# One transfer each for v, the sums and the reciprocals, a softmax chain spread over three periods, and finer waits into the second GEMM

## What is computed

```python
scores = cap * tanh((q @ k.T) / sqrt(64) / cap)      # batch 2, heads 12, seq 448, head_dim 64
attn = exp(scores - max) / (sum + 1e-9)
x = attn @ v                                         # then laid out as 896 x 768
h = x @ w_in                                         # 768 x 2048
x = maximum(0.01 * h, h) @ w_out                     # 2048 x 768
xn = x / rms(x) * rms_g
out = (silu(xn @ w_gate) * (xn @ w_val)) @ w_out2    # 768 x 1536, 1536 x 768
```

## Time and profile before

| | us |
|---|---|
| median of 3 runs | 644.47 (642.46 to 645.29) |
| the profiled execution | 639.19 |
| its span, first to last instruction | 637.1 |
| PE busy | 609.0 (96%) |
| DVE, POOL, ACT busy | 280.9, 203.8, 161.4 |
| mean granted clock of TensorE | 0.989 of full speed |

### The profile page before, as it was taken

The page is one execution under the profiler, slowest core; times in us unless marked ns, Lnnn a source line. Parts: engine busy times, 40 slices in busy tenths (PEclk is TensorE's granted clock), DMA queues, the critical chain, the costliest instruction groups (busy, mean ns, idle before and its releaser), DMA issues.

```text
span 637.1 us, 7470 instructions
## 1 busy us (share of the span) xinstructions
PE 609.0 (96%) x2988; PEld 529.8 (83%) x2988; DVE 280.9 (44%) x383; ACT 161.4 (25%) x227; POOL 203.8 (32%) x124
## 2 busy tenths in 40 slices
PE   4987999899999997999999999999999999999998
PEld 3543555389999996999999999999999999999998
DVE  3274655388888785033331236445434454110000
ACT  5773766223233231001111023112111111100000
POOL 1020000035445453144342343536454352332000
PEclk9997999899999998999999999999999999999999
DMA  6134343324333333021111121212221220023000
GB/s 202 36 86 106 77 121 89 90 70 124 99 118 107 103 121 108 34 66 34 67 56 36 50 74 48 77 50 75 54 95 51 74 74 1 26 75 125 37 26 37
DMA packets 33314, 47.76 MB, mean 75 GB/s; under 512 B 18176, under 2 KB 21504, under 8 KB 33280
## 3 DMA queue, kind: packets, MB, share of 16 engines
q1 hardware_dynamic: 33280, 47.29, 24.9%
HBM read 44.44 MB, written 2.80 MB: 74 GB/s over the span
## 4 chain that ended last, share of the span: by engine, by line
PE 91%; DVE 3%; issue 2%; ACT 2%; DMA 1%; POOL 1%; SPq 1%; DVEq 0%
PE ps L690 28%; PE ps L670 19%; PE ps L644 18%; PE ps L733 13%; PE ps L626 8%; PE ps L608 3%; PE ps L630 2%; PE ps L612 1%; ACT probs L355 1%; DVE g_lo L484 1%; DVE x_norm L460 1%; ACT probs L349 1%; DMA qk_raw<-in_qk 1%; POOL act_lo L322 0%; DVE qk_lo L435 0%
## 5 line engine op out<-in xcount | busy, mean ns | idle before, releaser
L297 POOL TENSOR_TENSOR w_lo<-w_raw,w_hi 128x768 fp32r<-128x768 f32 (+1 forms) x68 | 132.9, 1954 | 341.9 <-DVE w_hi L473 341.9
L473 DVE CAST w_hi<-w_raw 128x768 fp32r<-128x768 f32 (+1 forms) x68 | 39.5, 582 | 190.6 <-issue 128.2
L690 PE MATMUL ps<-x_hi,w_hi 128*128 128x448 f32 x288 | 82.0, 366 | 0.0
L690 PE MATMUL ps<-x_lo,w_hi 128*128 128x448 f32 x288 | 81.8, 365 | 0.0
L690 PE MATMUL ps<-x_hi,w_lo 128*128 128x448 f32 x288 | 81.8, 365 | 0.0
L626 PE MATMUL ps<-probs,v_ones 128*128 128x448 f32 x144 | 61.4, 579 | 10.4 <-issue 7.8
L644 PE MATMUL ps<-x_hi,w_hi 128*128 128x448 f32 x192 | 70.3, 366 | 0.5 <-POOL w_lo L297 0.5
L644 PE MATMUL ps<-x_lo,w_hi 128*128 128x448 f32 x192 | 70.1, 365 | 0.0
L644 PE MATMUL ps<-x_hi,w_lo 128*128 128x448 f32 x192 | 70.1, 365 | 0.0
L626 PEld LDWEIGHTS ps<-probs,v_ones 128*128 128x128 f32 x144 | 28.6, 204 | 38.8 <-issue 38.6
L484 DVE TENSOR_TENSOR g_lo<-g_full,g_hi 128x448 fp32r<-128x448 f32 x32 | 60.8, 1904 | 0.0
(11 more groups left out here) (84 smaller groups left out, 834.8 us busy)
## 6 DMA issues: line engine op xcount, KB each, us to landing
w_raw<-in_w_in SPq DMA_DIRECT2D x32, 384.0 KB, 3.0
w_raw<-in_w_out SPq DMA_DIRECT2D x12, 512.0 KB, 3.5
qk_raw<-in_qk SPq DMA_DIRECT2D x12, 480.0 KB, 4.3
w_raw<-in_w_gate SPq DMA_DIRECT2D x12, 384.0 KB, 3.0
w_raw<-in_w_val SPq DMA_DIRECT2D x12, 384.0 KB, 2.9
v_raw<-in_w_out SPq DMA_DIRECT2D x12, 384.0 KB, 3.0
recip_row<-recips SPq DMA_DIRECT2D x24, 112.0 KB, 2.9
v_ones<-in_v SPq DMA_DIRECT2D x24, 96.0 KB, 3.1
```

Source lines behind the costliest of these rows:

```text
L297: pool.tensor_tensor(w_lo[u % 2][:, 0:n], w_raw[u % 2][:, 0:n], w_hi[u % 2][:, 0:n].bitcast(F32), ALU.subtract).then_inc(w_lo_done, 1)
L473: dve.tensor_copy(w_hi[u % 2][:, 0:n], w_raw[u % 2][:, 0:n]).then_inc(w_hi_done, 1)
L690: last = pe.matmul(ps[:, 4 * fp + 2 * s + b, 0:S], w[s][:, c * 128:(c + 1) * 128], x[:, (b * KD + c) * S:(b * KD + c + 1) * S], start=(c = ...
```

## The change

**v, sums, reciprocals.** v lies in columns 0 to 63 of every block of `v_ones`, for both heads, and is loaded by one transfer a pair instead of four. The results of both heads then lie on partitions 0 to 63 and the sums of both on partitions 64 to 127. `keep_x` copies 65 partitions (64 of results and one of sums), one transfer spreads the sums of both heads, and one loads 64 partitions by 896 reciprocals. `normalise` reads both heads from partitions 0 to 63 and writes head 1 to partitions 64 to 127.

**The order.** In period p DVE does `split_qk(p + 2)`, `reciprocal(p - 1)`, `normalise(p - 2)` and then `keep_x(p)`. `normalise(10)` and `reciprocal(11)` stand behind `leaky(0)` of GEMM 1 and `normalise(11)` behind `g_lo(2)`. SP stores and loads back the reciprocals of pair p - 1 in period p, and v is loaded two pairs ahead.

**GEMM 2.** For the first output tile PE waits before each of the 16 blocks f for `g_lo` of that block, and no longer before the first block for the last but one.

The diff:

```diff
--- before.py
+++ after.py
@@ -77,7 +77,7 @@
         v_ones = [buf(f"v_ones{s}", (2 * MAIN + 1) * 128, F32) for s in range(2)]
         probs = [buf(f"probs{s}", (2 * MAIN + 1) * S, F32) for s in range(2)]
         x_raw = [buf(f"x_raw{s}", 2 * S, F32) for s in range(2)]
-        recip_row = [buf(f"recip_row{s}", S, F32) for s in range(2)]
+        recip_row = [buf(f"recip_row{s}", 2 * S, F32) for s in range(2)]
         x_norm = buf("x_norm", S, F32)
 
 
@@ -202,19 +202,14 @@
                 at_least(sp, pv_done, p - 1)
                 if p < 2:
                     sp.wait_ge(v_ones_set, p + 1)
-                for h in range(2):
-                    dst = tiles(v_ones[p % 2][:, h * MAIN * 128:(h + 1) * MAIN * 128], 128)[:, :, HEAD[h]]
-                    sp.dma_start(dst, v[p, :, h * MAIN:(h + 1) * MAIN]).then_inc(v_in[p % 2], 16)
-                    sp.dma_start(v_ones[p % 2][HEAD[h], 2 * MAIN * 128 + h * D:2 * MAIN * 128 + (h + 1) * D],
-                                 v[p, HEAD[h], 2 * MAIN]).then_inc(v_in[p % 2], 16)
+                sp.dma_start(tiles(v_ones[p % 2][:, :], 128)[:, :, 0:D], v[p]).then_inc(v_in[p % 2], 16)
 
             def spread_sums(p):
 
                 sp.wait_ge(x_raw_done, p + 1)
                 at_least(sp, eps_done, p - 1)
-                for h in range(2):
-                    row = x_raw[p % 2][D * (1 - h):D * (1 - h) + 1, cols(h)]
-                    sp.dma_start(sums[p % 2][HEAD[h], :], row.rearrange("o (p j) -> o p j", p=D)).then_inc(sums_in, 16)
+                sp.dma_start(sums[p % 2][:, :],
+                             x_raw[p % 2][D:D + 1, :].rearrange("o (p j) -> o p j", p=128)).then_inc(sums_in, 16)
 
             def store_recip(p):
                 sp.wait_ge(recip_done, p + 1)
@@ -224,9 +219,8 @@
 
                 sp.wait_ge(recip_out, 16 * (p + 1))
                 at_least(sp, x_norm_done, 2 * (p - 1))
-                for h in range(2):
-                    sp.dma_start(recip_row[p % 2][HEAD[h], :],
-                                 recips[p, cols(h)].partition_broadcast(D)).then_inc(recip_row_in[p % 2], 16)
+                sp.dma_start(recip_row[p % 2][HEAD[0], :],
+                             recips[p].partition_broadcast(D)).then_inc(recip_row_in[p % 2], 16)
 
             def load_w(src, u, n):
 
@@ -243,17 +237,22 @@
             load_w(w_in[0], 0, KD * 128)
             load_w(w_in[1], 1, KD * 128)
             load_qk(2)
+            load_v(1)
             for p in range(PAIRS):
+                if p > 0:
+                    store_recip(p - 1)
                 if p + 3 < PAIRS:
                     load_qk(p + 3)
-                if p + 1 < PAIRS:
-                    load_v(p + 1)
+                if p > 0:
+                    load_recip_row(p - 1)
+                if p + 2 < PAIRS:
+                    load_v(p + 2)
                 if p == PAIRS - 1:
                     load_w(w_in[2], 2, KD * 128)
                     load_w(w_in[3], 3, KD * 128)
                 spread_sums(p)
-                store_recip(p)
-                load_recip_row(p)
+            store_recip(PAIRS - 1)
+            load_recip_row(PAIRS - 1)
             for u in range(4, U_OUT):
                 load_w(w_in[u % N1], u, KD * 128)
             for m in range(KD):
@@ -439,12 +438,12 @@
 
                 dve.wait_ge(pv_done, p + 1)
                 at_least(dve, x_norm_done, 2 * (p - 1))
-                at_least(dve, sums_in, 32 * (p - 1))
-                dve.tensor_copy(tiles(x_raw[p % 2][:, :], S), ps[:, PV:PV + 2, 0:S]).then_inc(x_raw_done, 1)
+                at_least(dve, sums_in, 16 * (p - 1))
+                dve.tensor_copy(tiles(x_raw[p % 2][0:D + 1, :], S), ps[0:D + 1, PV:PV + 2, 0:S]).then_inc(x_raw_done, 1)
 
             def reciprocal(p):
 
-                dve.wait_ge(sums_in, 32 * (p + 1))
+                dve.wait_ge(sums_in, 16 * (p + 1))
                 at_least(dve, recip_done, p)
                 dve.scalar_tensor_tensor(sums_eps[:, :], sums[p % 2][:, :], 1e-9, sums[p % 2][:, :], ALU.mult,
                                          ALU.add).then_inc(eps_done, 1)
@@ -454,10 +453,10 @@
 
             def normalise(p):
 
-                dve.wait_ge(recip_row_in[p % 2], 32 * (p // 2 + 1))
+                dve.wait_ge(recip_row_in[p % 2], 16 * (p // 2 + 1))
                 at_least(dve, x_lo_done, p)
                 for h in range(2):
-                    dve.tensor_tensor(x_norm[HEAD[h], :], x_raw[p % 2][HEAD[h], cols(h)], recip_row[p % 2][HEAD[h], :],
+                    dve.tensor_tensor(x_norm[HEAD[h], :], x_raw[p % 2][HEAD[0], cols(h)], recip_row[p % 2][HEAD[0], cols(h)],
                                       ALU.mult).then_inc(x_norm_done, 1)
                 dve.wait_ge(x_norm_done, 2 * p + 2)
                 dve.tensor_copy(x_hi[:, cols(p)], x_norm[:, :]).then_inc(x_hi_done, 1)
@@ -502,19 +501,23 @@
             for p in range(PAIRS):
                 if p + 2 < PAIRS:
                     split_qk(p + 2)
-                keep_x(p)
                 if p == 2:
                     weight_hi(0, KD * 128)
                     weight_hi(1, KD * 128)
                 if p > 0:
-                    normalise(p - 1)
-                reciprocal(p)
+                    reciprocal(p - 1)
+                if p > 1:
+                    normalise(p - 2)
+                keep_x(p)
             for u in range(N1):
                 weight_hi(u + 2, KD * 128)
                 leaky(u)
                 if u > 0:
                     g_lo(u - 1)
-                if u == 1:
+                if u == 0:
+                    normalise(PAIRS - 2)
+                    reciprocal(PAIRS - 1)
+                if u == 3:
                     normalise(PAIRS - 1)
             dve.wait_ge(gains_in, 16)
             for b in range(B):
@@ -616,7 +619,7 @@
             def weigh(p):
 
                 pe.wait_ge(exp_done, 2 * p + 1)
-                pe.wait_ge(v_in[p % 2], 64 * (p // 2 + 1))
+                pe.wait_ge(v_in[p % 2], 16 * (p // 2 + 1))
                 at_least(pe, x_raw_done, p)
                 for t in range(MAIN):
                     if t == 2:
@@ -663,8 +666,8 @@
 
                     at_least(pe, y_done, 2 * m - 2)
                 for f in range(half * HALF_F, (half + 1) * HALF_F):
-                    if m == 0 and f in (0, N1 - 1):
-                        pe.wait_ge(g_lo_done, 2 * N1 - (f == 0))
+                    if m == 0:
+                        pe.wait_ge(g_lo_done, N1 + f + 1)
                     for w, g in ((w_hi, 0), (w_hi, 1), (w_lo, 0)):
                         for b in range(B):
                             last = pe.matmul(ps[:, 2 * (m % 2) + b, 0:S], w[half][:, (f % HALF_F) * 128:(f % HALF_F + 1) * 128],
```

## The result

| | us |
|---|---|
| before, median of 4 runs | 643.47 (641.95 to 645.29) |
| after, median of 4 runs | 620.03 (619.48 to 620.64) |
| ratio | 0.9635, 95% interval 0.9603 to 0.9666 |
| profiled execution, before and after | 639.19 and 620.48 |
| span of it, before and after | 637.1 and 618.7 |

The change makes the kernel 3.65% faster. The profiled execution, for which the sum was made, was forecast at 620.3 with a span of 618.2, and came out at 620.48 and 618.7.

What follows compares the result with a forecast made beforehand. PE was taken as the bound, losing time to waits and lower clock. Attention -16.4, GEMM 1 +2.6 and GEMM 2 -5.1 gave -18.9 us: profiled 620.3, plus 5.3 for the median, 625.6 us, range 620.5 to 631.0.

Steps and rivals of the forecast that it cites:

- The base: Whole kernel: the median of the runs would stay 5.3 us above the profiled execution, turning 620.3 into 625.6 us.
- More gained: 621.6 us: Rival, chance 0.12: about 4 us of extra waiting for v and `g_lo` in ordinary runs would go too.
- v in attention: Attention: PE waits for late v; loaded two pairs ahead it lands in time, and pairs take 8.12 us.
- Attention, sum: Attention as a whole: GEMM 1 would begin at 110.6 instead of 127.02 us, -16.4 us.
- Pair 2: Attention: DVE work caught under POOL delays `keep_x(2)`, so `weigh(3)` waits 0.35 us, between 0 and 0.8.
- Chain of the sums: Attention: sums, reciprocals and `normalise` stay hidden, with 2.3 us of slack on DVE and more for the load back.
- The rival that named the sums behind v: Attention, chance 0.07: sums queued behind v set the period once they land over 4.3 us after `keep_x`; 633 us.
- GEMM 1: First units of GEMM 1: moved DVE and SP work makes units 3, 4 and 6 wait, +2.6 us, between +0.5 and +5.
- The reading that each multiplication takes 2.2 us: GEMM 1: both multiplications of `normalise(10)` take 2.2 us whatever POOL does, costing 2 us more.
- The load of reciprocals: GEMM 1: if the merged load ran at half rate, 2.9 instead of 1.45 us, unit 4 would wait 1.45 longer.
- GEMM 2: Start of GEMM 2: the 3.84 us wait for `g_lo` and the lower clock behind it go, -5.1 us.
- The clock in GEMM 1: Rival, chance 0.25: the clock falls after the wait before unit 4, price 1.3 to 1.7 us; 627.2 us.

Runs made afterwards that it cites:

- e4: Kernel before with only the merged transfers of v, sums and reciprocals and the smaller `keep_x`, in the old order: 632.18 us, ratio 0.9877.
- e2: e4 with v also loaded two pairs ahead, without the spread over three periods or the finer waits of GEMM 2: 626.22 us, ratio 0.9785.
- e5: The changed kernel, unaltered, timed and traced again on another chip: 621.43 us, ratio 0.9682.
- e6: The changed kernel with the two coarse waits of GEMM 2 put back: 627.94 us.
- e13: The changed kernel, unaltered, timed and traced again beside e12: 620.65 us, ratio 0.9708.
- e12: The changed kernel without the spread of the sums' chain over three periods: 620.02 us, ratio 0.9707.

## Why the prediction was wrong, step by step

- **The base: wrong, and it decides.** The step that failed is the last line of the sum, from the profiled execution to the median "with the same difference", 5.3 us. After the change the median lies 0.5 us below its trace, not 5.3 above. The 5.3 came from three runs on one chip (642.46, 644.47, 645.29) beside a trace of 639.19. In the later groups the kernel before had medians of 639.64 to 640.56, 0.5 to 1.4 above that trace. So some 4 of the 5.3 us belonged to those three runs and not to the kernel, and what sets the runs of before apart is mostly the half clock (above), nearly all of which the change takes away. With a base 0.5 to 1.4 above the trace the same terms give 620.8 to 621.7 us, inside the range. Why the runs of before were some 3 us higher there is open: they have no trace and no clock on record.
- **The profiled execution: 620.3 forecast, 620.48 measured, in part by luck.** The terms miss by +0.7, +0.5 and -0.6 us and cancel. Two more traces of the changed kernel came out at 620.65 and 622.54.
- **"More gained: 621.6 us"** had a chance of 0.12, and its number came closer than the forecast. Its mechanism, 4 us of waits for v and for `g_lo` that vary from run to run, is shown only as far as the clock goes (above). Its range was added up wrongly too: 621.6 less 1.5 for the spread of the runs is 620.1, not 620.5, and with the lower bound of GEMM 1 (2.1 less than the sum) 618.0.
- **v in attention: right.** The landing times fitted, e4 and e2 take the waits away, and the pairs run at 8.10 us.
- **Attention, sum: -16.4 forecast, -15.7 measured** in the first trace and -16.5 to -16.8 in e5, e6 and e13. Pair 2 was 0.35 us in the forecast; it is a wait of 0.79 in the first trace, and some 0.2 in all in the others. The forecast had left out that a late landing of the sums also delays the next load of q and k. The multiplications under POOL took 2.6 us and not the 4.41 taken over from before, but the small reciprocal step was caught there too, 1.78 us instead of 0.17.
- **Chain of the sums: right that it is hidden (but for that place), wrong in its landing times.** Sums 1.9 forecast, 2.7 measured (2.2 in e5 and e13), load back 2.9 and 4.1. The rival that named the sums behind v had the direction and 3.3 us for it; the period would have had to wait for 4.3. The cross-partition multiplication cost nothing (0.619 us median), nor did `keep_x` on 65 partitions (1.09).
- **GEMM 1: +2.6 forecast, +3.1 measured**, at the three units named, for the reason named: SP's `load_w` at 10.95 us (11.35) behind the moved reciprocal. The landing of panel 4, taken at 3.3, was 4.1. The reading that each multiplication takes 2.2 us whatever POOL does falls: `normalise(10)` had 2.55 us for both. The load of reciprocals did not go at half rate. The first window of the earlier trace rows can't tell it, since a load of weights runs in it as well: 159 GB/s over 1.8 us are 286 KB, more than the 229 KB of the reciprocals. Where the load had the queue to itself it took 1.3 us, not 2.9 (changed kernel; us, POOL busy, clock, DMA share, GB/s):

```profile
102.80:104.10 1.30, 0.00 (x0) 1.00 0.54 176
```

  The Trainium skill, "SBUF — State Buffer", section "Can I just issue two DMAs to hit both halves?", says that two such transfers serialize, and this agrees with it.
- **GEMM 2: -5.1 forecast, -5.7 in the trace and -6.3 to -6.5 in medians.** The term that was too small is 13 matmuls at 0.203 us set against 3.90 us of the window: 1.24 us, where the two rows of the chain, 119.29 and 117.51, give 1.78.
- **The clock in GEMM 1: a rival with 0.25 that happens in eight executions of twelve,** if a mean clock of 0.997 is read as that fall, as the traces of e5 and e13 have it. The price was 1.6 us. That is what unit 4 pays, but some 0.7 come back at unit 6.
- **What was not priced by itself:** whether the spread over three periods brings anything. The working priced its loss in GEMM 1 and counted its gain with v's. By the traces it shortens attention by 0.7 to 1.7 us and lengthens GEMM 1 by 2.8 or more; in the medians of e12 and e13 nothing is left of it.

## What to carry to other kernels

Before a sum made on one trace is added to a median, ask how far the runs lie from that trace and whether the change takes away what sets them apart; keep both bases in the range. A second trace of the same kernel is as much needed: one wait of 0.8 us was there in one trace of four. A load that only needs a free buffer should not stand behind a chain of waits in an in-order queue: fewer transfers ahead of it were worth 8.4 us here and moving it ahead another 6.0, while spreading the chain behind it brought nothing by itself. When a step moves in one engine's program, follow what waits for it in the queues as well: here one late reciprocal held back the weight loads of the next stage.

## What the runs showed of the hardware

- A transfer of 3.5 KB issued 1.1 us behind one of 224 KB on the same queue lands after 2.2 to 2.7 us in the median of four traces (up to 4.6), against 1.9 for two of 1.8 KB with nothing ahead of them.
- One load of 64 partitions by 3.5 KB with the queue to itself took 1.30 us, 176 GB/s.
- VectorE multiplied from partitions 0 to 63 into partitions 64 to 127 in the same 0.62 us as within a half. A step on 7 elements took 1.78 us instead of 0.17 while GpSimd's subtraction ran.
- At the same place the granted clock fell after waits of TensorE of 2.34 and 2.37 us (0.57 from 128 to 132 us in the first) and stayed at full after 2.21 and 2.79.
- At a granted clock of 1.00 the same unit of 18 matmuls took 3.65 us in most traces and 3.72 in two; the cause is open.
